# A second order of steps for the last nine quarters of a fused three-stage kernel

## The reference, cut to what matters

```python
def _moe_ref(x, w_gate, w_val, w_out):            # first block, d_ff = 1536
    gate = 1.0 / (1.0 + np.exp(-(x @ w_gate)))
    val = x @ w_val
    return (gate * val @ w_out).astype(np.float32)

def _moe2_ref(x, w_in, w_out, a, b):              # second block, d_ff = 2048
    h = x @ w_in
    h2 = h * h
    h3 = h2 * h
    P = a[0] + a[1] * h + a[2] * h2 + a[3] * h3
    Q = 1.0 + np.abs(b[0]) * np.abs(h) + np.abs(b[1]) * h2
    g = P / (Q + 1e-06)
    return (g @ w_out).astype(np.float32)
```

## Time and profile before

| | us |
|---|---|
| median of 3 runs | 1393.13 (1392.23 to 1394.19) |
| profiled execution | 1391.3 |
| its span in the trace | 1389.5 |
| TensorE busy | 1351.8 (97%) |
| VectorE busy | 1247.1 (90%) |
| ScalarE busy | 1063.3 (77%) |
| GpSimd busy | 373.3 (27%) |

### The profile page before, as it was taken

How to read it: one execution, slowest core, us unless ns; L and a number is a source line. 1 busy time by engine, 2 the same in 40 slices (tenths; PEclk the granted TensorE clock), 3 DMA queues, 4 the chain that set the end, 5 groups by cost and what they waited for, 6 DMA issues and landing times.

```text
span 1389.5 us, 19167 instructions
## 1 busy us (share of the span) xinstructions
PE 1351.8 (97%) x7221; PEld 1223.9 (88%) x7221; DVE 1247.1 (90%) x1498; ACT 1063.3 (77%) x1452; POOL 373.3 (27%) x219
## 2 busy tenths in 40 slices
PE   5999999999999999999999999999999999999976
PEld 4899899999999999998999998998998998999966
DVE  7778999998998999999998998999999998889998
ACT  3487887777778787787778778778777778778975
POOL 0333233142332323233142333323233231210000
PEclk9999999999999999999999999999999999999999
DMA  9210100201011010200101011010100101000000
GB/s 241 75 48 17 52 16 14 61 1 59 16 41 34 1 59 16 59 16 22 53 1 59 16 40 35 0 59 17 57 17 32 40 1 50 16 14 22 13 8 18
DMA packets 48797, 49.09 MB, mean 35 GB/s; under 512 B 5696, under 2 KB 43074, under 8 KB 48704
## 3 DMA queue, kind: packets, MB, share of 16 engines
q1 hardware_dynamic: 48640, 47.85, 12.4%
q0 software_dynamic: 64, 0.00, 0.0%
HBM read 25.55 MB, written 6.29 MB: 23 GB/s over the span
## 4 chain that ended last, share of the span: by engine, by line
PE 90%; DVE 6%; issue 2%; ACT 2%; DMA 0%; SPq 0%; DVEq 0%
PE ring L361 49%; PE acc L390 39%; PE ring L416 1%; DVE work L764 1%; DVE work L785 1%; DVE work L758 1%; DVE work L778 1%; DVE work L771 1%; PE ring L419 1%; DVE work L794 0%; ACT work L543 0%; DVE work L701 0%; DMA window<-in_x_dram 0%; DVE u L752 0%; DVE val_w L718 0%
## 5 line engine op out<-in xcount | busy, mean ns | idle before, releaser
L390 PE MATMUL acc<-out_w,work 128*128 128x192 f32 x2048 | 363.5, 328 | 13.0 <-DVE work L794 13.0
L390 PEld LDWEIGHTS acc<-out_w,work 128*128 128x128 f32 x2048 | 339.8, 191 | 19.1 <-DVE work L794 13.2
L533 ACT ACTIVATE work<-ring,coef 128x512 f32<-128x512 f32 (+1 forms) x272 | 182.3, 670 | 223.1 <-PE ring L361 220.4
L361 PE MATMUL ring<-yt,in_w 128*128 128x512 f32 (+1 forms) x1360 | 325.3, 385 | 4.1 <-DVE work L764 2.0
L361 PEld LDWEIGHTS ring<-yt,in_w 128*128 128x128 f32 x1360 | 244.3, 188 | 49.5 <-DVE work L764 3.0
L390 PE MATMUL acc<-out_w,u 128*128 128x192 f32 x1536 | 283.0, 326 | 4.0 <-DVE u L752 3.8
L390 PEld LDWEIGHTS acc<-out_w,u 128*128 128x128 f32 x1536 | 255.5, 190 | 10.3 <-DVE u L752 3.9
L361 PE MATMUL ring<-xt,gate_w 128*128 128x512 f32 (+1 forms) x1020 | 262.1, 387 | 1.3 <-DVE val_w L718 0.8
L361 PE MATMUL ring<-xt,val_w 128*128 128x512 f32 (+1 forms) x1020 | 251.7, 377 | 0.0
L641 POOL TENSOR_TENSOR prod<-window,mixw 128x768 f32<-128x768 f32 (+1 forms) x90 | 135.3, 1503 | 399.1 <-DVE work L771 297.9
L361 PEld LDWEIGHTS ring<-xt,val_w 128*128 128x128 f32 x1020 | 185.0, 188 | 35.2
(11 more groups left out here) (61 smaller groups left out, 919.4 us busy)
## 6 DMA issues: line engine op xcount, KB each, us to landing
window<-in_x_dram SPq DMA_DIRECT2D x14, 960.0 KB, 4.7
yt<-ys SPq DMA_DIRECT2D x120, 64.0 KB, 2.0
xt<-xs SPq DMA_DIRECT2D x112, 64.0 KB, 2.0
out_dram<-zsb SPq DMA_DIRECT2D x15, 384.0 KB, 3.7
out_w<-in_moe_w_out_dram SPq DMA_DIRECT2D x1, 1536.0 KB, 19.4
mixw<-in_weight_gen_dram SPq DMA_DIRECT2D x13, 112.0 KB, 2.3
out_w<-in_moe_w_out_dram SPq DMA_DIRECT2D x2, 576.0 KB, 8.3
work<-in_moe_w_in_dram SPq DMA_DIRECT2D x2, 512.0 KB
```

The source lines that it names most:

```text
L361: last = nc.tensor.matmul(dst, wt[:, c], xs[:, 0:n], start=at == 0, stop=at == 4)
L390: last = nc.tensor.matmul(dst, src[:, n * P:(n + 1) * P], w[:, i, :], start=i == 0 and n % 2 == 0, stop=i == last_i and n % 2 == 1, skip_g ...
L533: nc.scalar.activation(den(n), h, ACT.Abs, scale=coef[:, 6:7])
```

## The change

A second string of letters, `TAIL_QUARTER`, holds from quarter `LAST` = 65 on (the second quarter of tile 16). ScalarE's and VectorE's loops stop before quarter 65, and a second loop with other lists of calls goes on from there. All calls, shapes and semaphores stay; GpSimd's and SyncE's lists are the same.

```diff
 QUARTER = "a1122bXYba221abb"
+
+TAIL_QUARTER = "a11222Xb2ab1abbY"
...
+    LAST = 4 * (NCH - 1) + 1
     def units(k):
 
-        return QUARTER.replace("X", "") + "X" if k == 3 else QUARTER
+        return TAIL_QUARTER if k >= LAST else QUARTER.replace("X", "") + "X" if k == 3 else QUARTER
...
-            for k in range(NK):
+            for k in range(LAST):
                 m, n, q = 3 * k, 4 * (k - OFF2), k - OFF2
...
+            for k in range(LAST, NK):
+                m, n, q = 3 * k, 4 * (k - OFF2), k - OFF2
+                if k % 4 == 0:
+                    y_copy(k // 4 - 1)
+                sigmoid(m)
+                rsqrt_squared(q - 1)
+                if (k - OFF2) % 4 == 2:
+                    z_copy((k - OFF2 - 2) // 4 - 1)
+                sigmoid(m + 1)
+                hidden(n)
+                hidden(n + 1)
+                hidden(n + 2)
+                hidden(n + 3)
+                if k % 4 == 0:
+                    y_high(k // 4 - 1)
+                sigmoid(m + 2)
+                rsqrt(q)
...
-            for k in range(NK):
+            for k in range(LAST):
                 m, n, p = 3 * k, 4 * (k - OFF2), 2 * (k - OFF2)
...
+            for k in range(LAST, NK):
+                m, n, p = 3 * k, 4 * (k - OFF2), 2 * (k - OFF2)
+                if k >= LAST + 1:
+                    quadratic(n - 3)
+                if k >= LAST + 1:
+                    denominator(p - 2)
+                if k >= LAST + 1:
+                    cubic(n - 3)
+                if k >= LAST + 1:
+                    quadratic(n - 2)
+                if k >= LAST + 1:
+                    denominator(p - 1)
+                if k >= LAST + 1:
+                    quadratic(n - 1)
+                if k >= LAST + 1:
+                    gated(m - 1)
+                if k >= LAST + 1 and k % 4 == 1:
+                    y_low((k - 1) // 4 - 1)
+                if k >= LAST + 1:
+                    cubic(n - 2)
+                if k >= LAST + 1:
+                    reciprocal(p - 4)
+                if k >= LAST + 1:
+                    cubic(n - 1)
+                if k >= LAST + 1:
+                    quotient(p - 4)
+                quotient(p - 3)
+                gated(m)
+                newton_product(p - 1)
+                newton_product(p - 2)
+                gated(m + 1)
+                quadratic(n)
+                reciprocal(p - 1)
+                cubic(n)
```

## The result

| | before | after |
|---|---|---|
| median | 1393.34 us (6 runs, 1392.23 to 1394.19) | 1388.92 us (6 runs, 1388.01 to 1389.56) |
| ratio to before | | 0.9968, 95% interval 0.9956 to 0.9981 |
| profiled execution | 1391.3 us, span 1389.5 | 1389.56 us, span 1387.8 |

The change takes 4.4 us off the median and 1.7 us off the two profiled executions.

A forecast was written before the change was run, and what follows sets the result against it. VectorE was taken to bound the tail. Pairs 2.88 plus waits for the square 1.08 less 0.6 at tile 16's input gave 3.36 us, so 1389.8 us against the median 1393.13; range 1388.3 to 1391.9.

The forecast's parts named there:

- VectorE is the bound of the tail, and only its holes can come back: From 1312.39 to its last instruction VectorE is busy 70.51 of 71.22 us; the order moves no work off it.
- Pairs: Quarters 65 to 72: two cubics and one quotient each, no longer right behind what they need, gain 2.88 us on VectorE.
- Without a price of a pair: Rival: VectorE's holes are filled otherwise, such as by a PSUM bank read; 0.5 us remain, 1392.6 us; chance 0.06.
- The rule quoted against the price: On VectorE the next operation waits until the pipe is empty anyway, so the 2.88 us would be nil: 1392.6 us.
- Waits for the square: VectorE's waits for rsqrt_squared, 0.19 us in quarter 66 and 0.89 in 67, both go; quarter 65's 0.19 stays: gain 1.08.
- The cover: VectorE has 6.1 us of other work during the 5.6 us from denominator to the square, so covered by 0.5 us.
- TensorE keeps pace at 15.45: In quarters 65 to 67 TensorE needs 15.3 us and follows VectorE at 15.45 instead of 15.96; 0.8 us kept for range.
- Tile 16's input: First step 4.7 us after y_low, 7.1 us idle, half clock some 3.4 us: loses 0.6, or 2.3 with twice the half clock.
- The end: TensorE's last b steps after VectorE's last quotient: none taken; 1.1 us back without half clock, up to 0.9 lost if longer.
- The sum is made for one execution and holds for the median: The 3.36 us, summed from the profiled execution of 1391.3 us, was also taken off the median 1393.13, giving 1389.8.
- the short covers: Rival: square chain, TensorE's pace and tile 16's input fall short; TensorE takes 0.8, input 1.7, leaving 2.1 us: 1391.0; chance 0.26.
- The slower case: Rival: tile 16's input comes too late, its first step some 6.8 us later at y + 11.5: 1396 us; chance 0.08.

The follow-up runs named there:

- two_pairs: The changed kernel with cubic(n - 3) and cubic(n) directly behind their quadratic again, the quotient left where it is; median 1391.3 us, ratio 0.9988 to the kernel before.
- vector_only: The kernel before with VectorE's new list from quarter 65 on, TensorE and ScalarE keeping their old lists to the end; median 1396.82 us, ratio 1.0029.
- early_input: The changed kernel with tile 16's input transposed early in quarter 68 through the first block's accumulator bank, no extra products; median 1387.56 us, ratio 0.9964 to the kernel before.

## Why the prediction was right, step by step

The forecast was 1389.8 us, the measured median 1388.92, in the lower part of its range. Against the median of 1393.13 that it started from that is 4.2 us, and 3.36 were forecast.

- *VectorE is the bound of the tail, and only its holes can come back.* Right. The rest of the tail was 102.1 to 102.4 us in every trace of the table.
- *Pairs: 24 times 0.12 us.* Right: 26 pairs (3.12 us) became 2 (0.24), and 16 put back cost 0.126 each. Without a price of a pair the two_pairs version would have had the tail of the new order without waits, and it was 2.01 us longer. The rule quoted against the price, from the Trainium skill ("VectorE: DVE Perf Modes", "The DRAIN you can't avoid"), was quoted in part. The same paragraph ends with "A next op that is not held starts earlier", and with that the starts 0.07 to 0.09 us before a listed end agree. The sentence that a semaphore "costs nothing extra here" was measured there on `tensor_copy`; for the instructions of this kernel the 0.126 us disagree.
- *Waits for the square: 1.08 us.* Right in size: 1.31 became 0.21, which is quarter 65's. The cover was thinner than the 0.5 us of the sum, which starts the chain at the end of `denominator`. In quarter 67 the root starts 0.37 us behind that end, because ScalarE's own table load is in front of it, and less than 0.2 us was left. With the root 0.95 us behind, in vector_only, 0.38 us of wait came back.
- *TensorE keeps pace at 15.45.* Right: the quarter took 15.35, and no VectorE wait came from it. (By the prediction's own terms the pace is 15.96 - 0.36 - 0.19 = 15.41.)
- *Tile 16's input: 0.6 us lost.* The way was right, with three waits of VectorE behind it where two were forecast. The first step came 4.59 us behind `y_low` (4.7 in the sum), after a pause of 7.12 (7.1). The size was wrong: 2.02 and 1.58 us in two traces. The term that was mis-sized is the 3.4 us of half clock. I took them from a stretch that began when TensorE began; here the clock had fallen during the pause, at about 1336.3, and was at half until 1346.5, 6.1 us behind TensorE's start (5.2 in the second trace). By my bound of twice the row it was 2.3.
- *The end: nothing.* Right. TensorE ended 2.56 us behind VectorE before and after, and 2.4 in the second trace after.
- *The sum is made for one execution and holds for the median.* This step failed in the other direction. 3.36 us was to be the difference of two executions and of two medians alike. Between the two profiled executions it was 1.7, as the input took 1.4 more than booked; the other 0.2 is the sum of small differences, some of them outside the tail. Between medians it was about 4, since the old order has waits at tile 16 in other executions (2.45 us in its second trace, about 1.5 in two more with extra products) and its first trace had none. The two misses nearly cancel, and 4.2 was measured for 3.36: that the sum came so near the medians is luck. That the profile was a favourable execution stood in the table: 1391.3 us, against 1392.23 to 1394.19 in the runs.

Of the rivals, the short covers came true in part: the input cost about what that case gave it (1.7; 2.02 and 1.58 were measured), but TensorE's pace cost nothing. The slower case did not come.

## What to carry to other kernels

Where one engine is full, look at starts and not at busy time: a VectorE step right behind its own input cost 0.12 us each time here, and another order gives it back for nothing, if that order also keeps each producer's bank or slot coming free when the other engines ask for it. A move of one instruction by one place lost 2.1 us, because that instruction was the release of a bank. Before a sum is made against one profile, compare its time with the spread of the runs, and ask which of its waits depends on a clock or a state that another execution can have otherwise. And where a pause is needed anyway, see what the engine does right behind it: seven idle microseconds cost 1.6 to 2 us here, in the traces that were taken, only through the clock, and small products in the pause, or the way round it, won those back.

## What the runs showed of the hardware

On VectorE an instruction that waited for the result of the one in front cost 0.126 us more than one that did not (16 pairs put together, 2.01 us).

TensorE's half clock lasted until 6.1, 5.2 and 2.8 us into its work after pauses of 7.12, 7.12 and 7.14 us in three traces, and until 3.8 us after one of 4.26, so the price of a pause isn't a constant. It also came behind pauses of 1.90 to 2.35 us in some traces, and at 1367.0 in early_input behind two of 0.86 and 0.80, while the first trace of before had a pause of 3.02 us at 1370.69 without it. The same code with the same pauses had it in one execution and not in another, or for 3.4 us in one and 6.8 in another.
